# Attention scores on a Trainium2 core: one 64-row product per head in place of block-diagonal pairs

## What is computed

```python
k_p = k.reshape(B, H, Sp, pool, D).mean(axis=3)      # 72 pooled keys a head
v_p = v.reshape(B, H, Sp, pool, D).mean(axis=3)
scores = scale * np.matmul(q, k_p.transpose(0, 1, 3, 2))
scores = scores - np.max(scores, axis=-1, keepdims=True)
attn = np.exp(scores)
attn = attn / (np.sum(attn, axis=-1, keepdims=True) + 1e-09)
x = np.matmul(attn, v_p)                             # to 4608 x 512
h = x @ w_in;  g = gate(h);  x = g @ w_out           # layer 1, 512 -> 2048 -> 512
h = x @ w_in2; g = h - tanh(h); y = g @ w_out2       # layer 2
```

## Time and profile before

| | us |
|---|---|
| median of three runs | 1693.8 |
| lowest and highest | 1693.38, 1695.77 |
| the profiled execution's own time | 1695.83 |
| its span, first to last instruction | 1694.1 |
| TensorE matmul busy in it | 1677.0 |
| VectorE, ScalarE, GpSimd busy | 733.5, 518.0, 187.3 |

### The profile page before, as it was taken

One profiled execution on the slowest core, in us unless ns is written; L12 is line 12 of the kernel. 1 busy time (PEld: TensorE's weight loads), 2 busy tenths in 40 slices (PEclk: granted clock), 3 DMA queues, 4 the chain that ended last, 5 costly groups with the idle time before them and its releaser, 6 DMA issues.

```text
span 1694.1 us, 17954 instructions
## 1 busy us (share of the span) xinstructions
PE 1677.0 (99%) x7684; PEld 1393.9 (82%) x7684; DVE 733.5 (43%) x1214; ACT 518.0 (31%) x913; POOL 187.3 (11%) x157
## 2 busy tenths in 40 slices
PE   6999999999999999999999999999999999999999
PEld 4888888888888888888888888888888888888887
DVE  6655655565555656455443323232232323232322
ACT  4533333333333333322343222222222222222222
POOL 5721102020111103001043000000000000000000
PEclk9999999999999999999999999999999999999999
DMA  9103020110302011010223010101010101010000
GB/s 341 66 1 115 0 88 28 50 66 1 115 0 88 29 50 38 0 50 1 75 100 124 1 50 0 50 0 50 0 50 0 50 1 50 0 50 1 25 1 25
DMA packets 28879, 77.69 MB, mean 46 GB/s; under 512 B 1408, under 2 KB 1408, under 8 KB 26752
## 3 DMA queue, kind: packets, MB, share of 16 engines
q1 hardware_dynamic: 28800, 76.55, 12.8%
HBM read 57.67 MB, written 18.87 MB: 45 GB/s over the span
## 4 chain that ended last, share of the span: by engine, by line
PE 98%; DMA 1%; POOL 0%; DVE 0%; ACT 0%; SPq 0%; issue 0%; POOLq 0%
PE acc_ps L466 46%; PE h_ps L458 33%; PE att_ps L458 7%; PE score_ps L458 6%; PE score_ps L509 1%; PE att_ps L488 1%; PE score_ps L488 1%; PE att_ps L500 1%; DMA v_raw<-v 1%; PE att_ps L509 0%; PE acc_ps L585 0%; PE score_ps L510 0%; POOL v_raw L402 0%; PE score_ps L500 0%; PE att_ps L510 0%; DVE probT_lo L854 0%
## 5 line engine op out<-in xcount | busy, mean ns | idle before, releaser
L466 PE MATMUL acc_ps<-g_hi,wout_hi 128*128 128x512 f32 x1152 | 449.7, 390 | 0.0
L466 PE MATMUL acc_ps<-g_hi,wout_lo 128*128 128x512 f32 x1152 | 448.8, 390 | 0.0
L466 PE MATMUL acc_ps<-g_lo,wout_hi 128*128 128x512 f32 x1152 | 448.7, 390 | 0.0
L458 PE MATMUL h_ps<-x_hi,win_hi 128*128 128x512 f32 x828 | 328.9, 397 | 0.0
L458 PE MATMUL h_ps<-x_hi,win_lo 128*128 128x512 f32 x828 | 323.2, 390 | 0.0
L458 PE MATMUL h_ps<-x_lo,win_hi 128*128 128x512 f32 x828 | 322.8, 390 | 0.0
L779 DVE TENSOR_TENSOR h_ps<-h_ps,bent 128x512 f32<-128x512 f32 x207 | 144.9, 700 | 295.6 <-ACT bent L627 208.7
L466 PEld LDWEIGHTS acc_ps<-g_hi,wout_lo 128*128 128x128 f32 x1152 | 216.4, 188 | 44.9
L466 PEld LDWEIGHTS acc_ps<-g_lo,wout_hi 128*128 128x128 f32 x1152 | 216.4, 188 | 44.4
L466 PEld LDWEIGHTS acc_ps<-g_hi,wout_hi 128*128 128x128 f32 x1152 | 216.4, 188 | 44.3
L768 DVE TENSOR_TENSOR g_lo<-h_ps,g_hi 128x512 fp32r<-128x512 f32 x207 | 142.9, 690 | 124.5 <-ACT g_hi L631 124.5
(11 more groups left out here) (127 smaller groups left out, 1478.5 us busy)
## 6 DMA issues: line engine op xcount, KB each, us to landing
stage<-kT SPq DMA_DIRECT2D x16, 576.0 KB, 4.7
x2T_scratch<-out_sb SPq DMA_DIRECT2D x9, 1024.0 KB, 4.2
x_lo<-x2T_scratch SPq DMA_DIRECT2D x9, 1024.0 KB, 7.3
win_raw<-w_in SPq DMA_DIRECT2D x8, 1024.0 KB, 8.8
wout_raw<-w_out SPq DMA_DIRECT2D x8, 1024.0 KB, 10.3
q_sb<-qT SPq DMA_DIRECT2D x8, 1024.0 KB, 4.9
yT<-out_sb SPq DMA_DIRECT2D x8, 1024.0 KB, 5.1
stage<-v SPq DMA_DIRECT2D x7, 1024.0 KB, 5.2
```

Of the source, the lines that this page charges most:

```text
L458: last = nc.tensor.matmul(h_bank(j, layer), w[:, c, j * P:(j + 1) * P], x_[:, c, :], start=(c == 0 and i == 0), stop=(c == KT - 1 and i == 2))
L466: last = nc.tensor.matmul(acc_ps[:, m, :], w[:, j, m * P:(m + 1) * P], g[:, j % GRING, :], start=(j == 0 and i == 0), stop=(j == FT - 1 an ...
```

## The change

Keys stay where the pooling puts them (`k_sum`, now with two buffers by batch). Each head's scores are a product of its own on 64 rows of the array, with 72 moving columns: even heads (g = 0) use partitions 0 to 63 and go to one bank, odd heads (g = 1) use partitions 64 to 127 and go to the other bank. The block diagonal, its memset, ScalarE's copies and the semaphore `k_pooled` are gone. Scores of a whole chunk are one call and wait for both groups of the chunk before. `prob` is laid out by pairs, so that a group's 4 x 72 elements are strided.

```diff
-KD_AT = STAGE_AT + max(KRAW, VRAW)
-VS_AT = KD_AT + 2 * PAIRS * 2 * KEYS
+KS_AT = STAGE_AT + max(KRAW, VRAW)
+VS_AT = KS_AT + 2 * PAIRS * KEYS
...
-        prob = at("prob", PROB_AT, [P, CHMAX, GROUPS, HG * KEYS])
+        prob = at("prob", PROB_AT, [P, CHMAX, PAIRS, 2 * KEYS])
...
+        def of_group(c, g):
+            return prob[:, c].rearrange("p a (e k) -> p a e k", e=2)[:, :, g, :]
...
-            def scores(n, k):
-                c, g = divmod(k, GROUPS)
-                if n == 0 and k == 0:
+            def scores(n, c):
+                if n == 0 and c == 0:
                     pe.wait_ge(q_first_loaded, 16)
-                if n == 0 and k < GROUPS:
-                    pe.wait_ge(k_pooled, k + 1)
-                if n == 0 and k == GROUPS * CHMAX // 2:
+                if n == 0 and c == 2:
                     pe.wait_ge(q_loaded, 16)
-                if n > 0 and k == 0:
+                if n > 0 and c == 0:
                     pe.wait_ge(q_loaded, 16 * (n + 1))
-                    pe.wait_ge(k_pooled, 2 * (min(n, BATCH - 1) + 1))
-                if n > 0 and k >= 2:
-
-                    pe.wait_ge(shift_done, GROUPS * before(n) + k - 1)
-                for row, rows, b in chunks(n)[c]:
-                    for e in range(2):
-                        p = 2 * g + e
-                        last = nc.tensor.matmul(score_bank(n, k)[row:row + rows, e * 2 * KEYS:(e + 1) * 2 * KEYS],
-                                                q_sb[:, c, p, row:row + rows], k_diag[:, b % 2, p, :],
-                                                start=True, stop=True)
-                last.then_inc(scores_done, 1)
+                    pe.wait_ge(k_reduced, 2 * (min(n, BATCH - 1) + 1))
+                if n > 0 and c >= 1:
+                    pe.wait_ge(shift_done, GROUPS * (before(n) + c))
+                for p in range(PAIRS):
+                    if n == 0 and c == 0 and p % 2 == 0:
+                        pe.wait_ge(k_reduced, p // 2 + 1)
+                    for row, rows, b in chunks(n)[c]:
+                        for g in range(GROUPS):
+                            own_rows = slice(g * DH, (g + 1) * DH)
+                            last = nc.tensor.matmul(
+                                score_bank(n, GROUPS * c + g)[row:row + rows, p * KEYS:(p + 1) * KEYS],
+                                q_sb[own_rows, c, p, row:row + rows], k_sum[own_rows, b % 2, p, :], start=True, stop=True)
+                            if p == PAIRS - 1 and row + rows == P:
+                                last.then_inc(scores_done, 1)
...
             def idle_products():
                 for _ in range(2):
-                    nc.tensor.matmul(sums[0], ident[:], k_diag[:, 0].rearrange("p a k -> p (a k)")[:, 0:T],
+                    nc.tensor.matmul(sums[0], ident[:], ident[:].unsqueeze(1).to_broadcast([P, T // P, P]),
                                      start=True, stop=True)
...
-            def place_k(b, half):
-                act.wait_ge(k_reduced, 2 * b + half + 1)
-                ...
-                last.then_inc(k_pooled, 1)
...
             def pool_k(b, half):
                 dve.wait_ge(k_loaded[half], 16 * (b + 1))
-                if b > 0:
-
-                    dve.wait_ge(k_pooled, 2 * (b - 1) + half + 1)
...
-                nc.vector.tensor_reduce(k_sum[:, cs], kr[:, cs], AX_X, ALU.add).then_inc(k_reduced, 1)
+                nc.vector.tensor_reduce(k_sum[:, b % 2, cs], kr[:, cs], AX_X, ALU.add).then_inc(k_reduced, 1)
...
-            nc.vector.memset(k_diag[:], 0.0).then_inc(zeroed, 1)
```

More of the change, by code:

```diff
@@ L119, in build @@
         ident = sb("ident", [P, P])
-        k_sum = sb("k_sum", [P, PAIRS, KEYS])
         own = sb("own", [P, 2])
@@ L146, in build @@
         stage = at("stage", STAGE_AT, [P, max(KRAW, VRAW)])
-        k_diag = at("k_diag", KD_AT, [P, 2, PAIRS, 2 * KEYS])
+        k_sum = at("k_sum", KS_AT, [P, 2, PAIRS, KEYS])
         v_sum = at("v_sum", VS_AT, [P, VTILES, DH])
         prob_tail = at("prob_tail", TAIL_AT, [P, CHMAX, 2 * PAIRS * TAIL])
-        prob = at("prob", PROB_AT, [P, CHMAX, GROUPS, HG * KEYS])
+        prob = at("prob", PROB_AT, [P, CHMAX, PAIRS, 2 * KEYS])
         out_sb = at("out_sb", OUT_AT, [P, KT, T])
@@ L174, in build @@
         k_reduced = sem("k_reduced")
-        k_pooled = sem("k_pooled")
         v_halved = sem("v_halved")
@@ L413, in normalise @@
                 pool.wait_ge(rcp_done, i)
-                tails = prob[:, c].rearrange("p g k -> p (g k)").rearrange("p (a r) -> p a r", r=PAIR_ROWS)[:, :, P:]
+                tails = prob[:, c, :, P:]
                 second = row_rcp[:, c, :].rearrange("p (a e) -> p a e", e=2)[:, :, 1]
@@ L422, in normalise @@
                 pool.wait_ge(tail_done, i)
-                pr = prob[:, c].rearrange("p g (h k) -> p (g h) k", k=KEYS)
+                pr = prob[:, c].rearrange("p a (e k) -> p (a e) k", k=KEYS)
                 nc.gpsimd.tensor_tensor(pr, pr, row_rcp[:, c, :].unsqueeze(2).to_broadcast([P, HEADS, KEYS]),
@@ L497, in turn @@
                     else:
-                        k = PAIR_ROWS * pair_of(i)
-                        cols = prob[:, c].rearrange("p g k -> p (g k)")[:, k:k + P]
+                        cols = prob[:, c, pair_of(i), 0:P]
                     last = nc.tensor.transpose(bank[:, c * P:(c + 1) * P], cols, ident[:])
@@ L515, in attention @@
                 if 0 <= s - 2 < len(chunks(n)):
-                    for g in range(GROUPS):
-                        scores(n, GROUPS * (s - 2) + g)
+                    scores(n, s - 2)
                 if s == 9:
@@ L576, in block_body @@
                     pe.wait_ge(acc_read_dve, 2 * blk + 2)
-            for k in range(GROUPS * len(chunks(0))):
-                scores(0, k)
+            for c in range(len(chunks(0))):
+                scores(0, c)
             h0, h1 = h_ps[:, 0], h_ps[:, 1]
@@ L642, in copy_sums @@
                     nc.scalar.copy(out_sb[:, m, :], acc_ps[:, m, :]).then_inc(acc_read_act, 1)
-            def place_k(b, half):
-                act.wait_ge(k_reduced, 2 * b + half + 1)
[L646 to L649, removed]
-                last.then_inc(k_pooled, 1)
             def exponent(n, c, g):
                 act.wait_ge(shift_done, GROUPS * (before(n) + c) + g + 1)
-                pr = prob[:, c, g, :]
+                pr = of_group(c, g)
                 nc.scalar.activation(pr, pr, ACT.Exp, scale=SCORE_SCALE).then_inc(exp_done, 1)
@@ L709, in block_body @@
                         nch = len(chunks(att))
-                        if s == 1 and att < BATCH:
-                            place_k(att, 0)
-                            place_k(att, 1)
                         if 0 <= s - 2 < nch:
@@ L726, in block_body @@
                         round_x2(blk + 1 - BLOCKS, s - 8)
-            place_k(0, 0)
-            place_k(0, 1)
             for c in range(len(chunks(0))):
@@ L823, in shift @@
                 dve.wait_ge(max_done, GROUPS * (before(n) + c) + g + 1)
-                nc.vector.tensor_tensor(prob[:, c, g, :].rearrange("p (h k) -> p h k", k=KEYS),
+                nc.vector.tensor_tensor(of_group(c, g),
                                         score_bank(n, GROUPS * c + g)[:, 0:HG * KEYS].rearrange("p (h k) -> p h k", k=KEYS),
@@ L830, in sum_rows @@
                 dve.wait_ge(exp_done, GROUPS * (before(n) + c + 1))
-                nc.vector.tensor_reduce(row_sum[:, c, :, 0], prob[:, c].rearrange("p g (h k) -> p (g h) k", k=KEYS),
+                nc.vector.tensor_reduce(row_sum[:, c, :, 0], prob[:, c].rearrange("p a (e k) -> p (a e) k", k=KEYS),
                                         AX_X, ALU.add).then_inc(sum_done, 1)
@@ L916, in block_body @@
                         split_x2(blk + 1 - BLOCKS, s - 8)
-            nc.vector.memset(k_diag[:], 0.0).then_inc(zeroed, 1)
             nc.vector.memset(row_sum[:, :, :, 1], 1e-9).then_inc(zeroed, 1)
-            dve.wait_ge(zeroed, 2)
+            dve.wait_ge(zeroed, 1)
             pool_k(0, 0)
```

## The result

The changed kernel takes 1700.53 us (median of 8 runs, 1699.57 to 1701.09), the kernel before 1694.79 us (8 runs, 1693.38 to 1696.98): ratio 1.003, 95% interval 1.0021 to 1.0038. It is 5.7 us slower; 1701 with a range of 1689 to 1729 was predicted. The profiled execution took 1700.78 us, its span is 1699.0.

A forecast was written before the change was run, and what follows sets the result against it. TensorE, busy 1677.0 of 1694.1 us, was taken to bound the kernel. Full chunks +9.0, split chunks -2.0 and the rest 0 gave +7.0 us on a median of 1693.8: 1700.8, say 1701 us, range 1689 to 1729.

The forecast's parts named there:

- The step from columns to rows: Scores on TensorE: row halves work at once, as column halves do in split chunks; lower bound 0.89 us, upper 1.78.
- rival 1: Full chunks: row halves take turns, 0.89 us more a chunk; about 1729 us, or 1718 without the switch price; chance 0.25.
- A record is bound by its load: Full chunks: loading 128 columns of weights, 0.11 us, sets a record's pace, not streaming 72 columns, 0.060 us.
- Rival 3: Score records: streaming alone sets the pace, 0.49 us a chunk; 1690 us with the switch, 1676 without; chance 0.06.
- The price of a visit: Full chunks: going into row halves and out is paid: 0.32 us to first load, 0.15 leaving, 0.34 to second large matmul.
- Rival 2: Chunks of scores: entering and leaving row halves costs nothing, so -6.4 us, 1687.5 us; chance 0.12.
- Rival 4: Full chunks: each alternation between halves costs a switch, seven a chunk at 0.15 us; +63 us, 1757 us; chance 0.05.
- Full chunk: 28 full chunks of the steady part: 1.76 us against 1.44, +0.32 each, +9.0 us in all.
- The narrower bounds 1695 and 1706: Total time, if the switch costs 0.15 us less or more a chunk and split chunks give -2.0 us or 0.
- Split chunk: Four split chunks: 1.35 us against 1.84, -0.49 each, -2.0 us if all four quarters work at once; 0 if not.
- Waits: VectorE's first maximum starts near 163.8 us instead of 163.22; 3.4 us of slack, so TensorE does not wait.
- Prologue: Start of the kernel: VectorE starts about 0.9 us later, covered by v's load; 0 to +0.1 us, clock 1 us either way.

The follow-up runs named there:

- e3: Changed kernel with each chunk's products issued all even heads first, then all odd heads; 1715.72 us, ratio 1.0119 to the kernel before.
- e2: Kernel before, with each pair's block-diagonal product cut in two of 72 moving columns, still on all 128 rows; 1723.82 us, ratio 1.0167.
- e1: Changed kernel with each chunk's 16 records made in two visits, before and behind the step's second_product; 1712.68 us, ratio 1.010 to the kernel before.
- e5: Kernel before with products per head on 64 rows in the four split chunks alone, full chunks keeping the block diagonal; 1693.3 us, ratio 0.9984.
- e7: Changed kernel with ScalarE's four copies a batch put back, into a tile that nobody reads; 1700.71 us against 1700.53 without them.
- e8: Changed kernel with every chunk in quarters (64 rows by 64 columns) and eight idle records in place of twelve; 1689.38 us, ratio 0.9962 to the kernel before.

## Why the prediction was right

- **Halves work side by side.** The step from columns to rows was the open one (rival 1 at 0.25). The pairs of starts show it, and e3 shows its condition, which the prediction did not have: I took any order to do. Had all even heads been issued ahead of the odd ones, the result would have been 1716 (e3), still inside the range but for a reason that I had not named.
- **A record is bound by its load.** 0.11 us predicted from the earlier trace rows, 0.11 measured with halves and 0.105 in e2 on all rows. The step that float32 weights load like fp32r ones held. Rival 3 falls.
- **The price of a visit.** Entering 0.32, the second large product 0.34, as taken from the earlier trace rows; e1 measures 0.35 us for a whole visit. Rival 2, a switch that costs nothing, falls. The page "TensorEngine Tiling (Array Packing)" of the Trainium skill, section Tiling Modes, has it drain; the trace agrees in that entering and leaving cost 0.35 us, while the starts show no price for going from one half to the other within a visit. Rival 4, a switch at each change of half, falls with the pairs.
- **Full chunk.** +0.32 predicted, +0.26 measured. What was too large is the term of the loads: I set eight whole loads behind the entering, 0.89, and 0.06 of streaming and 0.15 of leaving; from first to last start it is 0.84, and 0.20 to the next product. 28 x 0.06 = 1.7 us too much. From span to span the forecast's +7.0 becomes the measured +4.9 so: -1.8 for the full chunks, -0.1 for the split ones, +0.3 for the prologue, -0.5 for the large products behind the full chunks, at which the forecast didn't look.
- **The time itself.** 1701 was forecast and 1700.5 measured, and part of this nearness is luck: the forecast stood on a median of three runs, 1693.8, and eight runs of the same kernel gave 1694.8. The change was forecast 1.3 to 2.1 us too large, and the base was 1.0 us too low. The narrower bounds 1695 and 1706 don't follow from the two terms named there, which give 1696.6 and 1707.0; nothing hangs on them.
- **Split chunk.** 1.35 predicted, 1.32 measured; e5 gives -2.3 us for the four, where -2.0 stood in the sum.
- **Removed work.** Nothing predicted, nothing found for the copies of the steady part (e7).
- **Waits.** The first maximum comes later and TensorE doesn't wait; 3.8 us of slack where 3.4 were predicted. The maximum starts 1.46 us behind the last large product ahead of the scores, as predicted (163.8 - 162.31 = 1.49). VectorE's idling before it was put at 1.5 us and is 1.16, as its instruction before ends 0.3 us later against TensorE than in the kernel before.
- **Prologue.** 0 to +0.1 predicted, with 1 us either way for the clock; +0.3 found, in the idle products. The cover held, but only just: the first reciprocal ends at 18.19 us and GpSimd multiplies at 18.28. The difference is the clock, for which 1 us was allowed: I thought of when it falls, but here, by the spacing, it was low from the start to 23.2 us. The length of the idle records is read from one execution each, and it is not steady: the trace of e7, with the same TensorE program, has 7.28 us, so +0.3 is uncertain by as much.

## What to carry to other kernels

In this kernel, cutting a matmul into parts of the array paid only where the longer of load and streaming got shorter by it: halves of rows left 128 columns of weights to load (0.11 us a record), quarters did not (0.06). Each visit to halves between full-array products cost 0.35 us (e1), so few records a visit don't earn it. Issue the parts in turn: two records of each was the best order tried, four cost 0.05 us a chunk more, and with eight one part worked alone for 0.51 us.

## What was not expected

Three things. How few records may stand ahead of another half's: with four it starts at once, with eight 0.51 us late. That the large products behind the scores give back 0.02 us a chunk, which no term had; why was not tried. And the prologue of the changed kernel never reached the fast pace that the kernel before had from its third chunk on (12.8 us). Its records start 0.21 us apart until the last, at 15.7 us, which is twice the spacing of the steady part. The busy times by stretch of the changed kernel (columns as in the earlier trace rows) give the clock as 1.00 there:
```profile
12.80:16.30 3.50, 3.29 (x32) 3.08 (x30) 2.67 (x8) 1.33 (x3) 3.34 (x4) 1.00 1.05 396
```
The spacing and the loads of 330 ns contradict it, so at the start of an execution I go by the spacing. What makes the clock rise later here was not tried. How long TensorE stays slow in the prologue also goes with the spread of the kernel before: of its 18 executions beside e5 to e8, those with a mean granted clock of 1.000 have spans of 1692.1 to 1692.6 us and those with 0.998 have 1694.5 to 1695.7.
